# One slot's work in another order: masks moved between ratios and phases, ACT's angle and waves moved ahead of its gates

## The reference

```python
mag = np.sqrt(a_re * a_re + a_im * a_im)
scale = np.minimum(mag, 0.999) / (mag + 1e-06)
a_re_n, a_im_n = (a_re * scale, a_im * scale)
for t in range(S):                       # S = 768, per batch (4) and head (8), head_dim 48
    new_re = ar * S_re - ai * S_im
    new_im = ar * S_im + ai * S_re
    kv = np.einsum('bhd,bhe->bhde', k[:, :, t], v[:, :, t])
    S_re, S_im = (new_re + kv, new_im)
    y[:, :, t] = np.einsum('bhd,bhde->bhe', q[:, :, t], S_re)

h = x @ w_in;  g = h * np.clip(h + 3.0, 0.0, 6.0) / 6.0;                x = g @ w_out     # layer 1
h = x @ w_in;  g = np.maximum(h, 0.0) + alpha * np.minimum(h, 0.0);     x = g @ w_out     # layer 2
```

## Time and profile before

| | us |
|---|---|
| median of 3 runs (lowest to highest) | 1093.58 (1093.31 to 1095.88) |
| the profiled execution | 1091.72 |
| its span, first to last instruction | 1089.9 |
| PE busy | 971.5 (89%) |
| DVE busy | 700.0 (64%) |
| ACT busy | 487.9 (45%) |
| POOL busy | 304.5 (28%) |

### The profile page before, as it was taken

The page is one execution under the profiler, slowest core; times in us unless marked ns, Lnnn a source line. Parts: engine busy times, 40 slices in busy tenths (PEclk is TensorE's granted clock), DMA queues, the critical chain, the costliest instruction groups (busy, mean ns, idle before and its releaser), DMA issues.

```text
span 1089.9 us, 16711 instructions
## 1 busy us (share of the span) xinstructions
PE 971.5 (89%) x6178; PEld 952.6 (87%) x6178; DVE 700.0 (64%) x1234; ACT 487.9 (45%) x814; POOL 304.5 (28%) x291
## 2 busy tenths in 40 slices
PE   0156698699999999999999999999999999999998
PEld 0156687699998898989999999999999999999998
DVE  1884899799898898998989224553334344343432
ACT  2553766556766666667665345321212221221211
POOL 1222431122222222222221233333333333333332
PEclk9999899899999999999999999999999999999999
DMA  8353223333342332333323360101101010101000
GB/s 164 101 156 75 68 71 77 85 97 75 95 103 69 93 82 82 97 87 91 93 56 82 94 221 1 45 1 44 35 11 44 1 45 1 44 1 44 1 23 23
DMA packets 84803, 72.84 MB, mean 67 GB/s; under 512 B 34928, under 2 KB 80496, under 8 KB 84336
## 3 DMA queue, kind: packets, MB, share of 16 engines
q1 hardware_dynamic: 75120, 63.43, 21.3%
q10 hardware_dynamic: 9600, 8.33, 3.0%
HBM read 40.90 MB, written 9.44 MB: 46 GB/s over the span
## 4 chain that ended last, share of the span: by engine, by line
PE 55%; DVE 19%; ACT 8%; SPq 7%; issue 6%; DMA 4%; ACTq 1%; DVEq 0%
PE hp L1023 9%; PE op L1023 9%; PE hp L1025 9%; PE hp L1024 9%; PE op L1025 9%; PE op L1024 8%; SPq L358 3%; DVE t_phase L693 3%; DVE t_fb L728 3%; SPq L350 2%; ACT L515 2%; DMA wa_raw<-w_in 2%; DVE scores L747 2%; DVE t_inv L677 2%; DVE gated L775 2%
## 5 line engine op out<-in xcount | busy, mean ns | idle before, releaser
L465 POOL TENSOR_TENSOR g_lo<-gated,g_hi 128x384 fp32r<-128x384 f32 x256 | 270.1, 1055 | 693.2 <-ACT g_hi L554 693.1
L554 ACT ACTIVATE g_hi<-gated 128x384 fp32r<-128x384 f32 x256 | 133.6, 522 | 357.7 <-DVE gated L789 291.4
L785 DVE TENSOR_SCALAR gate<-hp,alpha_sb 128x384 f32<-128x384 f32 x128 | 79.1, 618 | 230.5 <-PE hp L1025 230.5
L1023 PE MATMUL hp<-x_parts,wa_hi 128*128 128x384 f32 x384 | 133.9, 349 | 19.4 <-DMA x_parts<-x_parts 18.0
L1023 PE MATMUL op<-g_hi,wb_hi 128*128 128x384 f32 x384 | 136.7, 356 | 9.4 <-ACT out_sb L559 8.6
L547 ACT ACTIVATE gate<-hp,half 128x384 f32<-128x384 f32 x128 | 73.7, 576 | 134.0 <-PE hp L1025 91.7
L1025 PE MATMUL op<-g_hi,wb_lo 128*128 128x384 f32 x384 | 130.9, 341 | 0.0
L1024 PE MATMUL hp<-x_parts,wa_hi 128*128 128x384 f32 x384 | 130.9, 341 | 0.0
L1024 PE MATMUL op<-g_lo,wb_hi 128*128 128x384 f32 x384 | 130.7, 340 | 0.0
L1025 PE MATMUL hp<-x_parts,wa_lo 128*128 128x384 f32 x384 | 130.6, 340 | 0.0
L1023 PE MATMUL op<-g_hi,wa_hi 128*128 128x384 f32 x384 | 129.9, 338 | 0.7 <-issue 0.7
(11 more groups left out here) (97 smaller groups left out, 1877.0 us busy)
## 6 DMA issues: line engine op xcount, KB each, us to landing
st<-prod SPq DMA_DIRECT2D x48, 145.1 KB, 3.1
st<-prod ACTq DMA_DIRECT2D x48, 145.1 KB, 2.9
a_sb<-a_in SPq DMA_DIRECT2D x24, 288.0 KB, 3.4
qk_sb<-qk_in SPq DMA_DIRECT2D x24, 288.0 KB, 3.5
v_pad<-v_in SPq DMA_DIRECT2D x24, 192.0 KB, 3.4
x<-out_sb SPq DMA_DIRECT2D x8, 576.0 KB, 3.2
x_raw<-x SPq DMA_DIRECT2D x8, 576.0 KB, 4.6
out<-out_sb SPq DMA_DIRECT2D x8, 576.0 KB, 3.2
```

The source lines that it names most:

```text
L465: pool.tensor_tensor(g_lo[:, at, :], gated[:, at * UT:(at + 1) * UT], g_hi[:, at, :].bitcast(F32), ALU.subtract).then_inc(glo_done, 1)
L554: act.activation(g_hi[:, at, :], gated[:, at * UT:(at + 1) * UT], ACT.Copy).then_inc(ghi_done, 1)
L785: dve.tensor_scalar(gate[:, at], hp[:, n % 2, 0:UT], 0.0, alpha_sb[:, m:m + 1], ALU.min, ALU.mult).then_inc(gate_done, 1)
L1023: pe.matmul(acc, lhs[0], rhs[0], start=start, stop=False)
```

## The change

No matmul and no DMA is added or taken away. On DVE the clamp of the ratios between -1.5 and 1.5 goes, with the semaphore behind it; all else is order:

- **DVE.** Position 0 was mags, phases, fractions, masks; it is mags, masks, phases, fractions, forward. Position 1 was forward, backward (with the product by q and k), products; it is backward, that product (now `factors`), x_low, products, state. x_low and state leave position 2. Of the three reciprocals one is now in position 2 and two in 3, none in 4.
- **ACT.** `angle` stands before the gate of position 0 and not behind it. `copy_k` of both halves and `waves` stand at the end of position 0; `waves` and one `copy_k` were behind the gate of position 1. `x_high` goes from position 2 to 1.
- **PE.** Both scores and `outputs`, `new_state` are in position 0. At the first item of a unit `hidden` comes before `output`.
- **SP.** `spread` before `stack`.
- **W_SPLITS.** No split in slot -2, four in each of slots -1 to 4.

```diff
-W_SPLITS = {-2: 3, -1: 3, 0: 3, 1: 3, 2: 4, 3: 4, 4: 4}
+W_SPLITS = {-1: 4, 0: 4, 1: 4, 2: 4, 3: 4, 4: 4}
 # SP, position 2
+                    if c0 is not None:
+                        spread(c0)
                     if c1 is not None:
                         stack(c1)
-                    if c0 is not None:
-                        spread(c0)
 # ACT
             def angle(c):
-                act.wait_ge(clamp_done, c + 1)
+                act.wait_ge(ratio_done, c + 1)
...
+                if pos == 0 and c1 is not None:
+                    angle(c1)
                 if n is not None:
                     gate_of(n + GSTEP)
-                if pos == 0 and c1 is not None:
-                    angle(c1)
-                if pos == 1 and c1 is not None:
-                    waves(c1)
-                if pos == 2 and c0 is not None:
+                if pos == 1 and c0 is not None:
                     x_high(c0)
                 if n is not None:
                     high(n + GSTEP)
-                if pos == 0 and keeps:
-                    copy_k(c0, 0)
-                if pos == 1:
+                if pos == 0:
                     if keeps:
+                        copy_k(c0, 0)
                         copy_k(c0, 1)
-                    if c2 is not None:
-                        magnitude(c2)
+                    if c1 is not None:
+                        waves(c1)
+                if pos == 1 and c2 is not None:
+                    magnitude(c2)
 # DVE
             def ratios(c):
...
-                dve.wait_ge(ratio_done, c + 1)
-                dve.tensor_scalar(flat(t_dt, 1), flat(t_dt, 1), 1.5, -1.5, ALU.min, ALU.max).then_inc(clamp_done, 1)
...
                     if c2 is not None:
                         mags(c2)
-                    if c1 is not None:
-                        phases(c1)
-                        fractions(c1)
                     if c0 is not None:
                         if c0 == 0:
                             dve.wait_ge(masks_set, 4)
                         mask(c0, 0)
                         mask(c0, 1)
-                if pos == 1 and c1 is not None:
-                    if c1 == 0:
-                        dve.wait_ge(pads_set, 3)
-                    forward(c1)
-                    backward(c1)
-                    products(c1)
-                if pos == 2:
+                    if c1 is not None:
+                        phases(c1)
+                        fractions(c1)
+                        if c1 == 0:
+                            dve.wait_ge(pads_set, 3)
+                        forward(c1)
+                if pos == 1:
+                    if c1 is not None:
+                        backward(c1)
+                        factors(c1)
                     if c0 is not None:
                         x_low(c0)
-                        if not is_last(c0):
-                            state(c0)
-                    if c2 is not None:
-                        clip(c2)
-                        numerators(c2)
+                    if c1 is not None:
+                        products(c1)
+                    if c0 is not None and not is_last(c0):
+                        state(c0)
+                if pos == 2 and c2 is not None:
+                    clip(c2)
+                    numerators(c2)
+                    inverse(c2, 0)
                 if pos == 3 and c2 is not None:
-                    inverse(c2, 0)
                     inverse(c2, 1)
+                    inverse(c2, 2)
                 if pos == 4 and c2 is not None:
-                    inverse(c2, 2)
                     ratios(c2)
 # PE
+            def first_half(n):
+                if n % MT_FF == 0 and n + HSTEP < 2 * N1:
+                    hidden(n + HSTEP)
+                else:
+                    output(n)
+            def second_half(n):
+                if n % MT_FF == 0:
+                    output(n)
+                elif n + HSTEP < 2 * N1:
+                    hidden(n + HSTEP)
...
                 if pos == 0 and c0 is not None:
                     score(c0, 0)
                     if keeps:
                         turn_k(c0, 0)
-                if n is not None:
-                    output(n)
-                if pos == 0 and c0 is not None:
                     score(c0, 1)
                 if n is not None:
-                    hidden(n + HSTEP)
+                    first_half(n)
                 if pos == 0 and keeps:
                     turn_k(c0, 1)
-                if pos == 1 and c0 is not None:
+                if n is not None:
+                    second_half(n)
+                if pos == 0 and c0 is not None:
                     outputs(c0)
```

More of the change, by code:

```diff
@@ L176, in build @@
         k_rows = sb("k_rows", [P, HEADS, ROWS2], F32, room)
-        ones = sb("ones", [P, CH], F32, room)
+        ones = sb("ones", [P, CH], F32, room)[:, :]
         causal = sb("causal", [P, CH], F32, room)
@@ L235, in build @@
         m2_done, worst_done, clip_done, inv_done = sem("m2_done"), sem("worst_done"), sem("clip_done"), sem("inv_done")
-        ratio_done, clamp_done, phase_done = sem("ratio_done"), sem("clamp_done"), sem("phase_done")
+        ratio_done, phase_done = sem("ratio_done"), sem("phase_done")
         whole_done, frac_done = sem("whole_done"), sem("frac_done")
@@ L692, in phases @@
                     start = 0.0 if is_first(c) else t_frac[:, 0, k, CH - 1:CH]
-                    scan = dve.tensor_tensor_scan(t_phase[:, 0, k, :], ones[:, :], t_dt[:, 1, k, :], start,
+                    scan = dve.tensor_tensor_scan(t_phase[:, 0, k, :], ones, t_dt[:, 1, k, :], start,
                                                   ALU.mult, ALU.add)
@@ L708, in forward @@
                 for k in range(KT_DM):
-                    scan = dve.tensor_tensor_scan(t_fb[:, 0, k, :], t_dt[:, 0, k, :], ones[:, :], 1.0,
+                    scan = dve.tensor_tensor_scan(t_fb[:, 0, k, :], t_dt[:, 0, k, :], ones, 1.0,
                                                   ALU.mult, ALU.mult)
@@ L730, in backward, with factors @@
                 scan.then_inc(back_done, 1)
+            def factors(c):
                 dve.wait_ge(qk_landed, 48 * (c + 1))
@@ L812, in _ @@
             dve.memset(tiny[:, :], 1e-6).then_inc(consts_set, 1)
-            dve.memset(ones[:, :], 1.0)
+            dve.memset(ones, 1.0)
             dve.memset(worst_all[:, :], -1e30)
@@ L1082, in _ @@
             for n in range(N_ATT, 2 * N1):
-                output(n)
-                if n + HSTEP < 2 * N1:
-                    hidden(n + HSTEP)
+                first_half(n)
+                second_half(n)
                 if n == N_ATT:
```

## The result

The changed kernel takes 1156.87 us (median of 4 runs, 1153.9 to 1160.12) against 1094.32 us (4 runs, 1093.31 to 1095.88): a ratio of 1.0571, 95% interval 1.0538 to 1.0604. Forecast were 1151 us. The span of the profiled execution is 1156.2 us against 1089.9 us, 66.3 us more.

A forecast was written before the change was run, and what follows sets the result against it. Before, PE and DVE were both near the bound; changed, DVE stalls on ACT's gates. +61 us in slots 7 to 23, 0 ahead and at unit starts, -4 at the end: 1149 us, median 1151 us; range 1130 to 1175.

The forecast's parts named there:

- The slots: Slots 7 to 23: DVE waits for ACT's gates at A, B and C; 465 us against 403.7 us, +61 us.
- A: Slot start, position 4 to 0: ACT's angle ahead of the gate; 5.0 us from gated to gated, DVE idles 3.0 us.
- B: Position 0 to 1: ACT's waves ahead of the gate; 9.0 us from gated to gated, DVE idles 1.9 us.
- C: Position 2 to 3: ACT's four stack DMAs ahead of the gate; 4.35 us from gated to gated, DVE idles 1.2 us.
- position 1 to 2: Part of a slot on DVE: 7.4 us, as before with one gated in it.
- only one of the stalls is real: Rival: A alone, or B and C alone, costs 3 us a slot instead of 6; about 1108 us, chance 0.09.
- Ahead of slot 7: First `hidden` 11 us early, at 93 us; slots 3 to 6 lose it again, slot 7 on time, 8 us either way.
- the 11 us of lead: First `hidden` at 93 instead of 104.23 us, as ACT no longer waits for the first weights; between 5 and 18 us.
- The end: From slot 24 on: PE waits for DVE there and is ahead by scores and an item, some 4 us less.
- At unit starts: PE's waits for output banks (8.6 us) and spread (18.0 us) go, worth 0 us as DVE's slot is longer.
- the rival of a falling clock: PE idles in pieces and its clock drops; decides below 0.81, at 0.75 gives 1190 us; chance 0.08.
- The table load: Rival: each table switch on ACT costs 2.66 us with a drain, 1.4 us more on A and B; 1199 us, chance 0.01.

The follow-up runs named there:

- experiment 1: Changed kernel with ACT's gate of position 0 ahead of the angle again: 1139.46 us.
- experiment 2: Changed kernel with ACT's waves back in position 1, behind the gate and ahead of `x_high`: 1126.55 us.
- experiment 7: Kernel before with only ACT's angle moved ahead of the gate of position 0: 1121.55 us.
- experiment 6: Changed kernel with only the stack put ahead of the spread on SP again: 1143.15 us.
- experiment 3: Changed kernel with the gate ahead of the angle and the waves behind the gate of position 1: 1109.58 us.
- experiment 4: As experiment 3, with `state` also back behind the gate of position 2 on DVE: 1108.1 us.
- experiment 10: As experiment 5, with PE's outputs and new_state back in position 1 and DVE's masks back behind phases and fractions: 1104.2 us.
- experiment 8: Kernel before with only the changed kernel's weight splits: 1084.61 us.
- experiment 12: Kernel before with the new splits, no clamp, and `hidden` ahead of `output` at a unit's first item (the best version): 1074.32 us.
- experiment 5: As experiment 4, with the stack also ahead of the spread on SP again: 1108.55 us.

## Why the prediction was right, point by point

- **The slots.** Right in mechanism; the size, +59.7 us in slots 7 to 23 against +61, is in part luck. In nearly every slot DVE waits by 3.5 to 3.7 us at A, by 2.0 to 2.6 us at B and by 0.8 to 1.9 us at C, each time on the gate behind the step that was named. Experiments 1, 2 and 7 move A and B by themselves and find both real; C was never tried alone. But 12.5 of the 59.7 us are the price of the spread ahead of the stack (experiment 6), a term that the sum doesn't have. Without it slots 7 to 23 took 450.9 us, +47 us: the sum's own terms were 14 us too large. Over the same ten slots the mean is then 26.4 us and not 27.4: position 1 to 2, put at 7.4 us, takes 6.7 us, and C, put at 4.35 us, takes 4.1 us. Two errors of about the same size met.
- **The pieces in slot 8.** A is 0.1 us longer than forecast, though the idle time there is 3.7 us and not 3.0, since ratios took 0.94 us instead of 1.49 and DVE was ready earlier. B is 0.5 us longer, since ACT's second `copy_k` waits 4.28 us for PE's transposes, which stand behind PE's matmuls at the lower clock level, and the waves start behind it; this holds in slots 7, 8 and 20. In the others the waves start with the fractions, as forecast, and the interval is 8.3 us in the seven of these with five items, where the forecast less its 0.5 us says 8.5 us. C is 0.4 us longer, since the four DMAs took 3.47 us and not 2.87.
- **The gate's loop is not alone.** The prediction left out that masks ahead of phases and spread ahead of stack close the loop D. At 25.2 us a slot in experiment 3, where A and B are gone, it lies below the 27.3 us (463.4 / 17) of a slot with A, B and C and so is partly hidden behind them; PE still waits 25.2 us for the stack between 205 and 670 us, and the spread's place costs 14 of the 63 us. Nor did it see that the outputs of position 0 come before `v`, which costs nothing that shows as long as a slot is this long. The same omission makes the rival "only one of the stalls is real" too cheap, and it is what failed in the expectations of experiments 1 to 4: the waits of one place were taken as time that comes back when they go, where the next limit stood some 2 us behind (27.3 - 25.2). With A alone left (experiment 2) it is 1127 us and with B alone left (experiment 1) 1139 us, where the rival said 1108.
- **Ahead of slot 7.** Mis-sized. The first `hidden` was forecast at 93 us and came at 99.24. The step that failed is the 11 us of lead: the first stack's lead was 10 us, and 8 us of it went in the slots to chunk 2, which took 22.4 and 23.1 us from score to score where before took 18.2 and 19.6. The 3.97 us of the spread in front of the stack explain a part only: with the stack first the two steps take 19.6 and 23.5 us, and the first `hidden` comes at 97.25 us. What makes the second step long in every version of the changed kernel (24.2 us in experiment 10, against 20.1 us in experiment 8) stays open. The rest, +10.9 us from the first `hidden` to slot 7, is what was forecast (18 - 1.6 - 5.3 = 11). Together slot 7 starts 5.9 us late instead of on time, within the 8 us given. With A undone, or B, it starts at 203.0 us, with both at 195.7 us.
- **The end.** "Ahead by scores and an item", -4 us, failed: from slot 24's gate to the end it is 484.1 us, before 483.4.
- **The sum.** 5.9 + 59.7 + 0.7 = 66.3 us; the 57 us forecast lack 5.9 and 4.7 and have 1.3 too much.
- **At unit starts.** Half right. The spread's wait went down from 18.0 to 8.2 us, all of it before 205 us, but the wait for the output banks is still 7.2 us: experiment 12 shows that the edit does take it away where ACT keeps its old order. That it is worth nothing in the changed kernel, as forecast, was not tried; on the order of before it is worth 4.7 us.
- **The clock.** In the stretch from 205 to 670 us the granted clock was 0.95, so the rival of a falling clock (below 0.81) didn't come about. PE was busy 88% and not 80% of it: the same work took 409 us where it had taken 389 us. But the mean hides the stretches of experiment 6, in which the clock was at its lower level of 1.2 GHz for all or a part of the time. PE had waited 1.8 to 3.5 us for the stack ahead of each of these eight, yet also 2.0 us in slot 12, where it stayed at 2.4 GHz. "TensorE: Matmul & The Clock Gate" (HAM oscillation) of the Trainium skill, by which such pieces put the clock back each time, is borne out in eight of 17 slots. What this did to the time (slower scores for which DVE waits, later transposes) can't be told apart here from the late stack itself.
- **The table load.** 1.28 us, with arctangent and copy 2.28 us from 262.48 to the gate at 264.76: the rival by "ScalarE: Activation LUTs" (What ACT_TABLE_LOAD costs) of the Trainium skill has no room, as forecast.
- **Of the gain and loss of the edits:** good are the splits (-9 us), the clamp (-6) and `hidden` first (-5), added one after the other to the order of before. Bad are A (-17 us when undone alone), B (-30) and the spread ahead of the stack (-14). Undoing the early masks gave 3 us, undoing the early outputs none that can be told, and `x_high` was not moved alone. Against the best version, experiment 10 still lacks 30 us: 5.7 at the first `hidden` (99.53 against 93.87), 9.2 from there to slot 8's first score, 15.4 from there to slot 24's. Which of the edits it still has (`x_high`, `x_low`, `copy_k`, `forward`, the second score, the reciprocals) costs how much stays open.

## What to carry to other kernels

A long step on one engine does most harm directly ahead of what another in-order engine waits for: put it behind the handed-over piece, not before. A wait that goes gives back only what lies between it and the next limit, so before counting a stall as gain, walk each loop from a result through all in-order queues back to itself (here scores, masks, phases, `x_low`, spread, stack, scores) and compare its length with the slot. And "earlier in the slot" is only earlier if the operands are there: outputs moved ahead of `v`, and `x_high` ahead of the outputs, each held what stood behind them in the traces. A forecast that hits should be opened as well: here two errors of 12 to 14 us in its largest term met, and only the run with one pair of lines exchanged on SP showed it.

## What was not expected of the hardware

- The issuing of the same DMAs varies within one kernel. ACT's four take 2.7 to 3.5 us in slots 7 to 23 of before and 2.7 to 3.9 us in the changed kernel; SP's eight take 5.93 us in slot 8 of before and 5.06 us in slot 9, and 5.00 and 6.44 us (4.50 + 1.94) in slots 7 and 8 of the changed kernel. It goes with how the two queues lie against each other: in eight of the nine slots of the changed kernel in which ACT's take 3.5 to 3.9 us, SP begins its stack 0.7 us after ACT; in the eight in which they take 2.7 to 2.9 us, SP begins its stack 1.1 to 2.6 us after. In experiment 6 SP begins 1.3 to 2.3 us ahead of ACT, and they take 2.7 to 2.9 us in all slots but one. Why was not tried.
- The same three scans over 128 columns take 1.94 us with POOL's low part beside them and 1.23 us without. The forecast bounded the gain at half of their time; it is 0.71 us at the phases. The backward scans have POOL's low part beside them in both kernels (1.95 us and 2.01 us); in slot 8 of experiment 5, without it, they take 1.22 us. The page "SBUF — State Buffer" (Who interferes with whom) of the Trainium skill is borne out by this pair.
- The first stack, 12 small DMAs issued by 28.3 us, landed at 38.9 us, while the weights were loading; in slot 8 the last was issued at 261.09 us and the scores began at 262.33 us.
